# A Fourier transform folded to 24 rows a frequency instead of 26, five frequencies to a group instead of four

## What is computed

```python
X = np.fft.fft(np.fft.fft(x, axis=1), axis=2).real          # per sequence
xk, xr = mu * x + (1 - mu) * x_prev                          # x_prev: the token before
r, v = sigmoid(xr @ w_r), relu(xk @ w_k) ** 2 @ w_v
x = r * v
expert = argmax(x @ w_gate); keep the first `capacity` tokens of each expert
out = gate * (relu(x @ w1[expert]) @ w2[expert])
```

## Time and profile before

| | us |
|---|---|
| median of three runs | 634.52 |
| the profiled execution, its own time | 635.9 |
| its span, first to last instruction | 634.1 |
| head, up to the first matmul of the tiles' `xr` products | 44.9 |
| an ordinary tile | 27.4 |
| tensor engine busy | 619.4 |
| vector engine busy | 448.1 |
| scalar engine busy | 324.8 |

### The profile page before, as it was taken

One profiled execution on the slowest core, in us unless ns is written; L12 is line 12 of the kernel. 1 busy time (PEld: TensorE's weight loads), 2 busy tenths in 40 slices (PEclk: granted clock), 3 DMA queues, 4 the chain that ended last, 5 costly groups with the idle time before them and its releaser, 6 DMA issues.

```text
span 634.1 us, 10636 instructions
## 1 busy us (share of the span) xinstructions
PE 619.4 (98%) x3474; PEld 531.1 (84%) x3474; DVE 448.1 (71%) x1020; ACT 324.8 (51%) x677; POOL 106.6 (17%) x105
## 2 busy tenths in 40 slices
PE   8989999999999999999999999999997999999995
PEld 5958888888888878887888888888885999999995
DVE  3568677978776687778877766778862777666671
ACT  1566445454545556545444546574543556655550
POOL 0530102020202011202010202020215011111111
PEclk9999999999999999999999999999998999999998
DMA  8947254251510023000000000050006545554100
GB/s 317 286 117 268 72 168 155 80 183 51 176 50 22 1 79 139 17 2 9 2 8 1 7 1 2 2 197 5 4 0 195 196 149 180 184 182 158 51 25 25
DMA packets 39596, 59.69 MB, mean 94 GB/s; under 512 B 4198, under 2 KB 31159, under 8 KB 39548
## 3 DMA queue, kind: packets, MB, share of 16 engines
q1 hardware_dynamic: 35708, 52.59, 25.4%
q0 software_dynamic: 3840, 6.52, 2.9%
HBM read 36.63 MB, written 26.91 MB: 100 GB/s over the span
## 4 chain that ended last, share of the span: by engine, by line
PE 95%; DVE 1%; DMA 1%; ACT 1%; issue 1%; POOL 0%; POOLq 0%; DVEq 0%; ACTq 0%
PE bank L292 76%; PE bank L1058 4%; PE bank L1003 3%; PE bank L1016 3%; PE bank L990 3%; PE bank L351 2%; PE bank L1392 1%; DMA got<-dispatched 1%; PE bank L1088 1%; PE bank L1401 0%; PE bank L1405 0%; PE bank L1402 0%; DMA dispatched<-rows,slot 0%; PE bank L1065 0%; POOL dispatched L510 0%
## 5 line engine op out<-in xcount | busy, mean ns | idle before, releaser
L292 PE MATMUL bank<-xk,wk 128*128 128x512 f32 x666 | 170.7, 400 | 0.0
L292 PE MATMUL bank<-k,wv 128*128 128x512 f32 x672 | 166.5, 398 | 0.0
L292 PEld LDWEIGHTS bank<-k,wv 128*128 128x128 f32 x672 | 125.9, 189 | 29.6
L292 PEld LDWEIGHTS bank<-xk,wk 128*128 128x128 f32 x666 | 123.4, 189 | 27.5
L621 ACT ACTIVATE relu<-bank 128x512 f32<-128x512 f32 x116 | 68.9, 596 | 114.6 <-PE bank L292 112.3
L510 POOL DMA_INDIRECT dispatched<-rows,slot x56 | 62.1, 1109 | 379.9 <-DVE slot L841 328.5
L859 DVE TENSOR_TENSOR square<-relu 128x512 f32<-128x512 f32 x116 | 80.1, 692 | 45.2 <-ACT relu L621 37.5
L854 DVE TENSOR_TENSOR k<-square,k 128x512 fp32r<-128x512 f32 x115 | 79.1, 688 | 2.8 <-ACT k L616 2.8
L616 ACT ACTIVATE k<-square 128x512 fp32r<-128x512 f32 x115 | 71.9, 625 | 9.9 <-DVE square L859 9.9
L292 PE MATMUL bank<-down_w,he 128*128 128x256 f32 x576 | 70.9, 284 | 0.0
L292 PEld LDWEIGHTS bank<-down_w,he 128*128 128x128 f32 x576 | 69.6, 192 | 0.0
(11 more groups left out here) (129 smaller groups left out, 748.3 us busy)
## 6 DMA issues: line engine op xcount, KB each, us to landing
out_rows<-blank SPq DMA_DIRECT2D x16, 768.0 KB, 4.0
raw_up<-in_moe_w SPq DMA_DIRECT2D x8, 1024.0 KB, 4.9
raw_down<-in_moe_w SPq DMA_DIRECT2D x8, 1024.0 KB, 8.5
x_area<-in_x SPq DMA_DIRECT2D x12, 512.0 KB, 5.7
dispatched<-blank SPq DMA_DIRECT2D x1, 3276.0 KB, 19.1
got<-dispatched SPq DMA_DIRECT2D x8, 409.5 KB, 3.0
y<-in_x SPq DMA_DIRECT2D x6, 512.0 KB, 7.4
first_partner<-in_x SPq DMA_DIRECT2D x2, 512.0 KB, 8.1
```

The costliest lines, as they stand in the source:

```text
L292: done = nc.tensor.matmul(bank, w, x, start=first and i == 0, stop=last and i == len(terms) - 1)
```

## The change

Residues 0 and 12 are their own reversals. Before, each had a row pair (cosine and sine part) like the other eleven, so a frequency had 2 x 13 = 26 rows. After, the real and the reversed input of these two are summed, and each has a single row: 2 x 11 + 2 = 24 rows a frequency. The two share one set of 256 channels in step 1 (set 11: residue 0's own 128 lower channels and residue 12's), so `x_own` has 12 sets instead of 13. One channel of each falls out of that scheme and is kept in a tile `apart` of two columns, made by one small DVE subtraction, and used by two small matmuls (one row, 65 columns) in step 1.

With 24 rows, five frequencies fit into 120 partitions. The frequencies 0 to 64 (now 65 of them) make 13 groups of five instead of 16 of four, so frequency 64 needs no treatment of its own. Step 1 has 24 matmuls of 130 columns and 2 small ones; steps 2 and 3 have 26 matmuls each instead of 32. The chunks of step 1 are 3, 3, 3 and 3 sets (before 4, 4, 4 and 1), the triples 3, 3, 3, 3 and 1 groups, and step 3 has groups of 4, 4, 4 and 1 (480, 480, 480 and 120 columns for each sum, before 4 x 384). What DMA loads for a sequence is 24 x 256 columns as before, in equal chunks.

```diff
-RESIDUES = [0, N2 // 2] + list(range(1, N2 // 2))
+RESIDUES = list(range(1, N2 // 2)) + [0, N2 // 2]
-JS = 4
-SG = (N1 // 2) // JS
-ROWS2 = 2 * NR * JS
+SETS = FOLDED + 1
+JS = 5
+JOWN = N1 // 2 + 1
+SG = JOWN // JS
+ROWS2 = N2 * JS
-CHUNKS = [(0, 4), (4, 8), (8, 12), (12, 13)]
-TRIPLES = [(0, 3), (3, 6), (6, 9), (9, 12), (12, 14), (14, 16)]
+CHUNKS = [(0, 3), (3, 6), (6, 9), (9, SETS)]
+TRIPLES = [(0, 3), (3, 6), (6, 9), (9, 12), (12, 13)]
+GROUPS3 = [(0, 4), (4, 8), (8, 12), (12, 13)]
...
-    first_quads, later_quads = [h_pair, r_pair, h_pair, r_pair], [r_pair, v_pair, r_pair, r_pair]
+    first_quads, later_quads = [r_pair, h_pair, r_pair, h_pair], [r_pair, v_pair, r_pair, r_pair]
...
+                    if c == len(CHUNKS) - 1:
+                        nc.scalar.activation(self_rows(1), of_self(far), ACT.Copy)
+                        far = far[:, 0:2 * (FOLDED - CHUNKS[c][0]) * JOWN]
                     nc.scalar.activation(far_copy[:, c % 2, 0:far.shape[-1]], far, ACT.Copy).then_inc(s1_far_copied, 1)
...
-                        if i >= 2:
-                            h, cols = WK_PIECES[i - 2]
+                        if i > 0:
+                            h, cols = WK_PIECES[i - 1]
...
+                    if hi == SETS:
+                        nc.vector.tensor_tensor(apart[:, :], x_own[:, FOLDED, 0:DIM:P], partner[:, FOLDED, 0:DIM:P], ALU.subtract).then_inc(apart_ready, 1)
+                        dve.wait_ge(apart_ready, seq + 1)
...
+                    if c == len(CHUNKS) - 1:
+                        nc.vector.tensor_copy(self_rows(0), of_self(bank))
                     nc.vector.tensor_tensor(s1_summed(c, 0), near, far, ALU.add)
...
+                            if a == FOLDED:
+                                done = mm(bank[0:1, at + JOWN:at + 2 * JOWN], apart[:, i:i + 1], c_first[:, residue, 0:JOWN], start=True, stop=True)
...
                     for j in range(JS):
-                        mm(edge_bank[0:N2, j:N1 // 2:JS], m_even[1][:, j:SCOLS:JS], last_k, start=True, stop=True)
-                    mm(edge_bank[0:N2, 0:1], m_even[0][:, 0:SCOLS:JS], last_k[:, 0:1], start=True, stop=True)
-                    mm(edge_bank[0:N2, N1 // 2:N1 // 2 + 1], m_even[0][:, SCOLS:SPECIAL], last_k[:, 0:1], start=True, stop=True).then_inc(edge_full, 1)
+                        done = mm(edge_bank[0:N2, j:JOWN:JS], m_even[:, j:SCOLS:JS], last_k, start=True, stop=True)
+                    done.then_inc(edge_full, 1)
```

More of the change, by code:

```diff
@@ L47 @@
 ROW = 2 * SPLIT + 1
-C3_COLS = 2 * SCOLS + 2 * SPECIAL
+C3_COLS = 2 * SCOLS
 FAR = float(1 << 20)
@@ L92, in constants @@
     return {
-        "c_first": f(first.reshape(N1, NR, 2, SG, JS).transpose(0, 1, 3, 2, 4).reshape(N1, NR * P)),
+        "c_first": f(first.reshape(N1, NR * 2 * JOWN)),
         "c_second": f(second),
@@ L554, in mirrors @@
                         act.wait_ge(s3_summed, DH * (QUADS * seq + g) + h + 1)
-                        if g == 0:
-                            nc.scalar.activation(mirror(1 - h, 1, JS), by_s(h)[:, :, 1:JS], ACT.Copy)
-                            last = nc.scalar.activation(mirror(1 - h, JS, QUAD * JS).rearrange("p s (i j) -> p i s j", j=JS),
-                                                        by_s(h)[:, :, JS:QUAD * JS].rearrange("p s (i j) -> p i s j", j=JS), ACT.Copy)
-                        else:
-                            last = nc.scalar.activation(mirror_quad(1 - h, g), straight(h, g), ACT.Copy)
+                        lo, hi = mirrored_js(g)
+                        last = nc.scalar.activation(mirror(1 - h, lo, hi), by_s(h)[:, :, lo:hi], ACT.Copy)
                         last.then_inc(s3_mirrored, 1)
@@ L564, in edge_out @@
                     act.wait_ge(edge_full, seq + 1)
-                    nc.scalar.activation(edge[:, :], edge_bank[0:N2, 0:N1 // 2 + 1], ACT.Copy).then_inc(edge_drained, 1)
+                    nc.scalar.activation(edge[:, :], edge_bank[0:N2, 0:JOWN], ACT.Copy).then_inc(edge_drained, 1)
                 def slot0(h, lo, hi):
@@ L987, in step1 @@
                     near, far = s1_banks(pairs, c)
-                    for bank, channels, full1 in ((far, slice(P, DIM), s1_far_full), (near, slice(0, P), s1_near_full)):
+                    for i, bank, full1 in ((1, far, s1_far_full), (0, near, s1_near_full)):
                         for a in range(lo, hi):
-                            done = mm(bank[:, (a - lo) * P:(a - lo + 1) * P], x_own[:, a, channels], c_first[:, a, :], start=True, stop=True)
+                            at = 2 * (a - lo) * JOWN
+                            residue = a + i if a == FOLDED else a
+                            done = mm(bank[:, at:at + 2 * JOWN], x_own[:, a, i * P:(i + 1) * P], c_first[:, residue, :], start=True, stop=True)
+                            if a == FOLDED:
+                                done = mm(bank[0:1, at + JOWN:at + 2 * JOWN], apart[:, i:i + 1], c_first[:, residue, 0:JOWN], start=True, stop=True)
                         done.then_inc(full1, 1)
@@ L1012, in step3 @@
                     for bank, lo, m, full3 in ((odd, 0, m_odd, s3_odd_full), (even, ZO, m_even, s3_even_full)):
-                        for i in range(QUAD):
-                            q = QUAD * (g + 1) - 1 - i
-                            moving = m[min(q, 1)]
-                            done = mm(bank[:, i * SCOLS:i * SCOLS + moving.shape[-1]], z[:, q, lo:lo + P], moving, start=True, stop=True)
+                        for q in range(*GROUPS3[g]):
+                            at = (q - GROUPS3[g][0]) * SCOLS
+                            done = mm(bank[:, at:at + SCOLS], z[:, q, lo:lo + P], m, start=True, stop=True)
                         done.then_inc(full3, 1)
```

114 lines of the change are left out of this document (53 added, 61 removed).

## The result

| | us |
|---|---|
| before, median of four runs | 634.70 (634.38 to 634.90) |
| changed kernel, median of four runs | 629.06 (628.74 to 630.32) |
| ratio, 95% interval | 0.9915 (0.9898 to 0.9933) |
| forecast | 628.4, range 626.8 to 630.8 |

A forecast was written before the change was run, and what follows sets the result against it. TensorE was taken to bound the kernel, with 95% of the chain. Two later transforms -5.0, tile 2 +0.47 and the head -1.6 sum to -6.1 us, so 634.52 becomes 628.4, range 626.8 to 630.8.

The forecast's parts named there:

- The price of a pass: TensorE's steps 1 to 3: 0.111 us for 130 or 120 moving columns, between bounds 0.110 and 0.116.
- step 2: Later transforms' step 2 on TensorE: 12 passes fewer at 0.1095 each, -1.31 us per transform.
- The rule of moving columns: Rival: passes cost by moving columns, so step 3 gains nothing; -3.2 us in all, 631.3; chance 0.06.
- Step 1: Later transforms: four long passes fewer save 0.44 us, four small ones add 0.30 (0.24 to 0.44); net -0.14.
- The wait in step 3: Tiles 5 and 11: last group waits for DVE's sums, 0.3 us new wait in each (0.1 to 0.7).
- Tile 2: DVE's longer `pair` additions and the subtraction into `apart` make TensorE wait 0.47 us more.
- The head: First transform: step 2's start within 0.3 of 19.14, step 3 1.05 earlier, slot 0 0.6 more; -1.6 us (-0.8 to -2.0).
- The edge's DMA: Head: must land before ACT's second patch; landing 37.7 against a need at 37.5, at worst some tenths late.
- The clock rival: TensorE's clock falls in the head as gaps grow by 1.0 us; costs 2.5, so -3.6, 630.9; chance 0.05.
- everything moves as a block: Second phase and its hand-over were taken to move as a block, with no term of their own.

The follow-up runs named there:

- e_half_moving: Changed kernel, step 3 of later transforms moving 60 of 120 columns per matmul; 600.94 us for a shorter program, tiles 5 and 11 at 35.55.
- e_half_still: Changed kernel, step 3 of later transforms with 64 of 128 stationary columns; 602.73 us, ending after fewer tiles, tiles 5 and 11 at 35.98 and 35.96.
- e_late: Changed kernel with step 1's two small matmuls together at the end of the last chunk; 629.21 us in one run.
- e_noapart: Changed kernel without the two small step 1 matmuls on `apart`; 627.12 us in one run.
- e_order: Changed kernel, last `pair` behind `gate_out` and low parts in tiles 2, 8; second group's mirrors after relu in tiles 5, 11; median 629.93 us, ratio 0.9915.
- e_sem: Kernel before the change with one unused semaphore added; 636.47 us in one run.
- c_after: Changed kernel run again unchanged; median of six runs 629.44 us, ratio 0.9922 to the kernel before.
- c_before: Kernel before the change, run again unchanged; 636.59 us in one run.
- e_best_late: Changed kernel with later `pair` (tiles 2, 8), relu ahead of edge, mirrors and copy (tiles 5, 11), small step 1 matmuls together last; 628.39 us, ratio 0.9895.
- e_layout: Changed kernel with two unused tiles restoring the earlier addresses of weights and tile operands; median 629.57 us, ratio 0.9911.
- e_wide: Changed kernel whose two small step 1 matmuls take 128 stationary columns instead of one; 628.58 us in one run.
- e_shift: Kernel before with one unused semaphore, which TensorE counts up 45 times at the start; 640.62 us.

## Why the prediction came out as it did

**The price of a pass and step 2** were right: 0.110 and -1.27 for -1.31. The rule of moving columns, one of the rivals, is refuted by `e_half_moving`: half of them gave 0.05 us a tile and not 2.9. The reason that I set against it, that the stationary side is what is paid for, is refuted by `e_half_still`: with half of the stationary columns the pass stayed at 0.111. My number stood on the row, and held; its reason did not. By the Trainium skill ("TensorE: Matmul & The Clock Gate", "LDWEIGHTS (loading the stationary operand)") a load's time follows the stationary columns; the time of a pass did not.

**Step 1** was mis-sized: -0.14 forecast, +0.39 and +0.46 found. I priced the four small passes by interpolation between short and long ones, 0.08 each, 0.30 in all, and kept 0.44 as the upper end. They cost 0.80, beyond the bound. 0.40 of it are the passes, 0.10 each (0.08 where they follow each other, in `e_late`). What I left out is the return from a narrow to a full stationary operand, 0.2 each. It was to be had in the trace of before, in the chain right behind the earlier trace rows:

```profile
393.01 1.96 PE bank L1016 x16
```

against 1.76 for the same 16 passes ahead of the edge. I counted the edge's own passes and not what stood behind them. In two tiles that is 1.1 us. In the head `e_noapart` reaches step 2 10.98 us after the start of step 1, where the changed kernel takes 11.57, so there they cost 0.6.

**The wait in step 3**: 0.3 forecast, 0.28 found, released by DVE's sums as said. Its parts grew by less than I had, 0.15 for two mirrors, 0.06 for the copy and 0.15 for two sums (0.20, 0.08 and 0.20 forecast). `e_order` shows that the order on ACT mattered as well: relu, square, low half and sums stand behind the copy in turn. With the relu ahead the tiles became 0.37 shorter, more than the wait of 0.28: without it the group also holds TensorE for 0.37 instead of 0.44.

**Tile 2**: +0.47 forecast, +0.49 found, and shown by removing it.

**The head**: -1.6 forecast, -0.9 to -1.0 found from the start of step 1 (35.94 against 36.82 and 36.96; `e_sem`, the kernel before but for a semaphore, has 37.39), within the range of -0.8 to -2.0. Step 2's start moved +0.35 instead of 0, by the small matmuls (without them, in `e_noapart`, it is 0.24 earlier than before); step 2 gave -0.82 for the -1.05; from step 3 to slot 0 it was 9.38 for the 9.35 forecast. The edge's DMA was in time: slot 0's second patch still follows the `xk` copy. But the bound on it is real. `e_noapart` starts on slot 0 26.78 after step 1's start, 0.6 sooner, and still reaches the first `xr` product after 35.92: DVE's `difference` ran beside GpSimd and took 0.32 longer, and ACT waited for the edge's DMA before the second patch. So the small matmuls by themselves do not account for the 0.6 that I missed.

**Not in the prediction**: the ordinary tiles' 0.11 us, 1.5 us over 14 tiles. It made good most of what step 1 lost (1.1) and the head fell short (0.6). Without it the time would have been near 630.5, still in the range. It is a property of the kernel, and its cause is open. That the total fell so near the forecast is therefore luck.

**The clock rival** did not happen in the head: from 36 to 45 us the granted clock was 1.00 in the changed kernel's profile too. But it happened where I had taken for granted that everything moves as a block. From the last `route_rows` to the end it took 167.3 before and 165.3 after, though nothing there was changed, and 165.4 to 167.3 in the other profiles that ran all 14 tiles, of either kernel. Nearly all of this lies in one stretch, from the first matmul on `got` (the tokens that the first expert gets) to its first `down`. Windows of that stretch before, in the changed kernel's first profile, and in `c_after` (with an earlier stretch ahead of it) were:

```profile
484.51:496.25 11.74, 11.49 (x61) 10.98 (x61) 4.92 (x9) 4.84 (x11) 4.66 (x2) 0.85 0.97 336
```

```profile
479.20:489.55 10.35, 10.10 (x61) 9.54 (x61) 4.92 (x9) 4.84 (x11) 5.31 (x3) 1.00 0.88 315
```

```profile
474.50:477.90 3.40, 3.40 (x6) 1.67 (x6) 0.00 (x0) 1.29 (x2) 0.00 (x0) 0.50 0.56 161
479.17:489.48 10.31, 10.06 (x60) 9.50 (x61) 4.93 (x9) 4.83 (x11) 6.71 (x4) 1.00 0.79 262
```

Ahead of that stretch TensorE stands still, in the profile of before for 1.73 us ahead of extra matmuls and for 2.42 us until the DMA of `got` lands, and in nine of the twelve profiles its clock then falls to 1.2 GHz once. Where it falls within the stretch, the granted clock is 0.85 over it, and it takes 11.36 to 11.74 us (the kernel before, `c_before`, `e_sem`, `e_late`, `e_order`, `e_best_late`). Where it falls earlier, during extra matmuls (`c_after`, `e_layout`, `e_wide`), or not at all (the changed kernel's first profile, `e_noapart`, `e_shift`), the stretch takes 10.29 to 10.35. So the fall costs 1.0 to 1.4 us there or nothing, by when it comes, and in both kernels alike. From the last `route_rows` to that stretch it is 16.99 to 17.76, without such an order, and what follows the stretch takes 137.81 to 137.87 in every profile.

This is why the profiled spans differ by 6.7 us (634.1 and 627.4): the tiles gave 5.09, the head 1.02 and the second phase 2.03, and the start took back 1.42. The tiles and the head alone make 6.1. The medians say 5.6, and 5.0 for `c_after` (629.44 against 634.46), with both scatters in them.

## What to carry to other kernels

Count what stands behind a small matmul, not only the matmul: with a stationary operand of 1, 24 or 64 columns the next full one starts about 0.2 us late, and a full operand for the same 65 columns was cheaper. When work is packed into fewer and larger groups, follow the chain that frees the banks for the next group: each stage grows by the ratio, and here a slack of 0.17 us became a wait of 0.28, which went away when ACT's relu, whose input was there already, was put ahead of the larger copies. And where TensorE is the bound everywhere, compare tile by tile and not total by total: the tiles repeat to 0.03 us, the totals only to 1 or 2, and most of that scatter was TensorE's clock, at the start and at the hand-over to the second phase.

## What was not expected of the hardware

- A matmul of 128 rows, one stationary and 65 moving columns in fp32 costs 0.1 us a pass and, ahead of a full stationary operand, 0.2 us behind it; with 128 stationary columns 0.11 and nothing.
- Passes of fp32 took 0.108 with 60 moving and 128 stationary columns, 0.111 with 120 and 64, 0.111 with 120 and 128, 0.110 with 129 and 120.
- DVE's subtraction of 512 columns took 1.01 to 1.18 us instead of 0.69 when it started about half a microsecond before GpSimd's long subtraction ended.
- The extra matmuls at the start ended between 7.8 and 9.4 us, as TensorE went from half to full clock between 4.90 and 8.10 us; the view shows 1.00 for the half clock ahead of it.
- One fall of the clock to 1.2 GHz at the hand-over to the second phase cost 1.0 to 1.4 us where it met the first expert's matmuls, and nothing in that stretch where it came during extra matmuls.
